# Spare products of ones and the identity at the start of a windowed attention, and masks made in two parts

## The reference, cut to what is computed

```python
def _attn_ref(q, k, v, n_global, n_local):          # q, k, v: 4 x 8 x 768 x 64
    scores = scale * np.matmul(q, k.transpose(0, 1, 3, 2))
    is_global = pos[None, :] < int(n_global)         # 8
    is_local = (rel >= 0) & (rel < int(n_local))     # 96
    dist = np.where(is_global & ~is_local, float(n_local), np.abs(rel))
    scores = scores - slopes[:, None, None] * dist   # a slope per head
    scores = np.where(is_global | is_local, scores, -1e9)
    a = softmax(scores)
    return np.matmul(a, v)
```

## Time and profile before

| what | us |
|---|---|
| median of three runs | 505.05 (504.94 to 505.18) |
| the profiled execution's own time | 504.66 |
| span of its instructions, first to last | 502.9 |
| TensorE busy | 479.9, or 95% of the span |
| VectorE busy | 363.8, or 72% |
| ScalarE busy | 346.6, or 69% |
| GpSimd busy | 94.4, or 19% |

### The profile page before, as it was taken

The page is one execution under the profiler, slowest core; times in us unless marked ns, Lnnn a source line. Parts: engine busy times, 40 slices in busy tenths (PEclk is TensorE's granted clock), DMA queues, the critical chain, the costliest instruction groups (busy, mean ns, idle before and its releaser), DMA issues.

```text
span 502.9 us, 12848 instructions
## 1 busy us (share of the span) xinstructions
PE 479.9 (95%) x4604; PEld 398.6 (79%) x4604; DVE 363.8 (72%) x1026; ACT 346.6 (69%) x763; POOL 94.4 (19%) x223
## 2 busy tenths in 40 slices
PE   2999999999999998998899999999999999999996
PEld 1667777677676642426689999999999999999996
DVE  5687877786787571318998978777587777768782
ACT  2788897887888710008999877777777776777740
POOL 1545554554455404400000000000000000000000
PEclk9999999999999999999999999999999999999999
DMA  7699889885565789994001011010110101001011
GB/s 284 256 343 366 343 316 328 322 299 195 175 200 195 296 327 405 417 404 162 1 1 44 2 43 42 0 42 0 42 42 0 42 0 42 28 14 42 0 43 42
DMA packets 17979, 77.24 MB, mean 154 GB/s; under 512 B 2320, under 2 KB 2320, under 8 KB 14352
## 3 DMA queue, kind: packets, MB, share of 16 engines
q1 hardware_dynamic: 14720, 60.95, 32.8%
q10 hardware_dynamic: 3216, 15.73, 8.2%
HBM read 70.39 MB, written 6.29 MB: 152 GB/s over the span
## 4 chain that ended last, share of the span: by engine, by line
PE 76%; ACT 9%; DVE 4%; DMA 3%; issue 3%; SPq 2%; POOL 1%; DVEq 0%; ACTq 0%; POOLq 0%
PE bank L1652 14%; PE bank L1651 14%; PE bank L1653 14%; PE bank L1308 5%; ACT probs L1028 5%; PE bank L1623 4%; PE bank L1296 4%; PE bank L1323 4%; DMA w_a<-w_dram 2%; PE bank L1328 2%; SPq L413 2%; PE bank L1291 2%; PE bank L1369 2%; PE bank L1580 2%; PE bank L1348 2%
## 5 line engine op out<-in xcount | busy, mean ns | idle before, releaser
L1028 ACT ACTIVATE probs<-probs,nmax 128x232 f32<-128x232 f32 (+1 forms) x192 | 88.6, 463 | 31.1 <-DVE nmax L554 30.2
L464 POOL TENSOR_SCALAR probs<-probs,rden 128x232 f32<-128x232 f32 (+1 forms) x192 | 82.5, 448 | 89.0 <-DVE rden L563 89.0
L1651 PE MATMUL bank<-t_hi,s_hi 128*128 128x256 f32 x352 | 98.7, 280 | 0.0
L1652 PE MATMUL bank<-t_lo,s_hi 128*128 128x256 f32 x352 | 98.6, 280 | 0.0
L1653 PE MATMUL bank<-t_hi,s_lo 128*128 128x256 f32 x352 | 98.5, 280 | 0.0
L1151 ACT ACTIVATE g_s<-bank 128x1024 f32<-128x1024 f32 x47 | 47.9, 1022 | 29.2 <-PE bank L1623 29.2
L1199 ACT ACTIVATE s_hi<-s 128x512 fp32r<-128x512 f32 x88 | 55.0, 627 | 18.5 <-DVE s L956 14.7
L1651 PEld LDWEIGHTS bank<-t_hi,s_hi 128*128 128x128 f32 x352 | 66.5, 189 | 0.0
L1652 PEld LDWEIGHTS bank<-t_lo,s_hi 128*128 128x128 f32 x352 | 66.4, 189 | 0.0
L1653 PEld LDWEIGHTS bank<-t_hi,s_lo 128*128 128x128 f32 x352 | 66.4, 189 | 0.0
L879 DVE TENSOR_TENSOR s_lo<-s,s_hi 128x512 fp32r<-128x512 f32 x88 | 56.9, 687 | 6.8 <-DVE s L956 3.5
(11 more groups left out here) (200 smaller groups left out, 1024.2 us busy)
## 6 DMA issues: line engine op xcount, KB each, us to landing
qkv_s<-qkv_dram SPq DMA_DIRECT2D x15, 1028.0 KB, 7.3
qkv_s<-qkv_dram SPq DMA_DIRECT2D x16, 704.0 KB, 5.9
w_s<-w_dram ACTq DMA_DIRECT2D x5, 2048.0 KB, 11.4
w_s<-w_dram SPq DMA_DIRECT2D x13, 512.0 KB, 8.6
out_dram<-o_stage SPq DMA_DIRECT2D x24, 256.0 KB, 2.0
wo_raw<-w_out_dram SPq DMA_DIRECT2D x4, 1024.0 KB, 14.5
w_a<-w_dram SPq DMA_DIRECT2D x3, 1024.0 KB, 11.6
w_a<-w_dram SPq DMA_DIRECT2D x5, 512.0 KB, 7.5
```

The lines of the kernel that those rows point to most:

```text
L464: last = pool.tensor_scalar(probs[:, v % 2, m, a, 0:w], probs[:, v % 2, m, a, 0:w], rden[:, v % 2, m, a:a + 1], 1.0, ALU.mult, ALU.mult)
L1028: act.activation(probs[:, v % 2, m, a, 0:w], probs[:, v % 2, m, a, 0:w], ACT.Exp, bias=nmax[:, v % 2, m, a:a + 1], scale=-1.0, accum_out=d ...
L1651: pe.matmul(OUT[n], hi, W_HI[n](at_f), start=(c == 0 and f == 0 and n in (0, 2, 4, 5)), stop=False, skip_group_check=True)
L1652: pe.matmul(OUT[n], hi, W_LO[n](at_f), start=False, stop=False, skip_group_check=True)
```

## The change

The first tile's masks of heads 0 and 1 are made as soon as the first tile's tables stand, and `bias_scores(0, 0)` is split: tile `m` = 0 is masked before the tables and masks of the other tiles are made, tile `m` = 1 after. The masks of later heads move by one step: those of head s + 1 are made after step s, for s from 1 to 6. TensorE gets products of `ones` and `ident` into a part of bank 7 that nobody reads: 12 before its step 0 (after a wait for the identity, which before stood behind step 0), 4 behind step 0 and 22 behind step 1.

```diff
-                own(dve.tensor_scalar(drop[:, at_g], col[:, 0:GLOB], ng, masked, ALU.is_ge, ALU.mult))
-                own(dve.scalar_tensor_tensor(drop[:, :], rel[:, :], nl, drop[:, :], ALU.is_ge, ALU.mult))
-                own(dve.tensor_scalar(dist[:, :], rel[:, :], nl, None, ALU.min))
-
-                def make_bias(h):
+
+                def make_bias0(h):
 
                     slope = 2.0 ** (-8.0 * (h + 1) / HEADS)
                     dve.scalar_tensor_tensor(bias0_of(h), dist0[:, :], -slope / SCALE, drop0[:, :], ALU.mult, ALU.add)\
                         .then_inc(masks_ready, 1)
+
+                def make_bias(h):
+
+                    slope = 2.0 ** (-8.0 * (h + 1) / HEADS)
                     dve.scalar_tensor_tensor(bias_of(h), dist[:, :], -slope / SCALE, drop[:, :], ALU.mult, ALU.add)\
                         .then_inc(masks_ready, 1)
 
-                for h in range(2):
-                    make_bias(h)
-
-                def bias_scores(b, v):
+                def bias_scores(b, v, tiles=(0, 1)):
                     p, i0 = divmod(2 * v, TILES)
-                    for m in range(2):
+                    for m in tiles:
...
-                for s in range(STEPS):
-
-                    dve.wait_ge(masks_ready, 2 * min(s + 2, HEADS))
+                for h in range(2):
+                    make_bias0(h)
+                dve.wait_ge(masks_ready, 2)
+                bias_scores(0, 0, (0,))
+                own(dve.tensor_scalar(drop[:, at_g], col[:, 0:GLOB], ng, masked, ALU.is_ge, ALU.mult))
+                own(dve.scalar_tensor_tensor(drop[:, :], rel[:, :], nl, drop[:, :], ALU.is_ge, ALU.mult))
+                own(dve.tensor_scalar(dist[:, :], rel[:, :], nl, None, ALU.min))
+                for h in range(2):
+                    make_bias(h)
+                dve.wait_ge(masks_ready, 4)
+                bias_scores(0, 0, (1,))
+                recips(0, 0)
+                for s in range(1, STEPS):
+                    dve.wait_ge(masks_ready, 2 * min(s + 1, HEADS))
                     step(0, s, False)
-                    if s + 2 < HEADS:
-                        make_bias(s + 2)
+                    if s + 1 < HEADS:
+                        make_bias0(s + 1)
+                        make_bias(s + 1)
...
+            def idle_start(n):
+
+                for _ in range(n):
+                    pe.matmul(bank[7][:, 0:P], ones[:, :], ident[:, :])
+
             if windowed:
+                pe.wait_ge(iotas, 6)
+                idle_start(12)
                 for s in range(STEPS):
                     step(0, s, False)
-                    if s == 0:
-                        pe.wait_ge(iotas, 6)
+                    if s < 2:
+                        idle_start((4, 22)[s])
```

## The result

The changed kernel takes 511.67 us (median of 6 runs, 511.27 to 513.75) against 505.12 (504.81 to 505.88) for the kernel before: a ratio of 1.0139, 95% interval 1.0127 to 1.0152. The medians are 6.55 us apart. The profiled execution took 511.46, its span 509.7 against 502.9, so 6.8 us of difference are there to be read. The forecast was 509.7 with a range of 507.8 to 512.8. The direction and the range held. The place of the loss was the one named, but the likeliest case, with its own range of 508.9 to 510.5, was not the one that came: TensorE's clock fell after the gap, the rival given 0.25. The range held because it had been drawn wide enough for that rival.

The account below looks back on a forecast made before the run. At the start, whichever engine each step waits for bounds the kernel: TensorE for step 2, then VectorE's loop. 4.5 us (step 2) plus 0.15 (later masks) gives 4.7, so 509.3 profiled, 509.7 median; range 507.8 to 512.8.

Parts of the forecast that it names:

- the likeliest case: The main forecast, chance 0.58: TensorE's clock stays up and the time is 509.7 us, own range 508.9 to 510.5.
- the rival given 0.25: TensorE's clock falls while idle between step 1's scores and step 0's transposes: 1.9 to 2.8 us more, 511.6 to 512.5.
- Part 1, the 12 products: Ahead of step 0: 24 records from 2.40 us, clock rising at 7.3, hold up the scores; tile 0 masked at 8.4.
- Part 2, the masks: Step 0 on VectorE: other tiles' tables and masks stand behind the wait for TensorE; sums arrive at 12.4 against 11.38.
- d: Delay of step 0's sums from the held-up scores and new mask order: 1.1 us, bounds 0.65 to 2.0.
- Part 3, the 4 products: Behind step 0 on TensorE: 0.9 us fast or 1.7 slow, hidden because VectorE wants step 1's scores only at 12.9.
- Part 4, the 22 products: Between step 0's transposes and step 2's scores: 44 records, 4.9 us; step 2 masked at 21.4, 4.5 us late.
- the two bursts: TensorE work from 5.26 and 12.89 us in the kernel before, read as bounding the clock's rise to 3.9 to 5.9 us.
- Part 5, later masks: Step 6 gains a pair of masks, step 0 loses one: 0.15 us before step 7, bounds 0 and 0.35.
- The products did not pass the waiting transposes: Rival, chance 0.08: TensorE runs the 22 products in the gap, ahead of the waiting transposes: 503.8 to 504.8 us.
- Nothing was taken up later: Rival, chance 0.04: a wait in the loop hides the delay, time within 0.2% of 505.05 us.
- The clock did rise early: Rival, chance 0.05, claimed the opposite: first products too little to raise the clock, d 2.0, 22 products slow: 512.9 us.

Follow-up runs that it names:

- masks_alone: The changed kernel with its new mask order and none of the added products: 504.66 us, ratio 0.9999 to the kernel before.
- no_22: The changed kernel without the 22 products behind step 1: 505.90 us, ratio 1.0016 to the kernel before.
- only_22: The kernel before, old masks, with only the 22 products behind step 1 added: 510.45 us, ratio 1.0112 to the kernel before.
- twice_22: The changed kernel with 44 products in place of 22 behind step 1: 516.22 us, ratio 1.0220 to the kernel before.
- gap_filled: The changed kernel with 12 more products between step 1's scores and step 0's transposes: 508.98 us, ratio 1.0088 to the kernel before.
- old_masks_12_4: The kernel before, old masks, with 12 products ahead of step 0 and 4 behind it: 504.54 us, ratio 0.9992.
- fill_old: The kernel before, old masks, with 10 products ahead of step 0, 4 behind it, 8 before step 0's transposes: 504.53 us, ratio 0.9986.
- fill_new: The changed kernel with 8 products ahead of step 0, 4 behind it, 12 before step 0's transposes, no 22: 504.38 us, ratio 0.9983.

## Why the prediction was right, and where it was off

Step 2 was to come at 21.4 and came at 23.53; the sum to there was 4.5 and is 6.63.

- **Part 1, the 12 products.** Right, and late within its bounds. The steps were 0.213 us and the last of the 24 records began at 7.48, but the scores began only at 7.83: 0.35 us after the last product's start where a step of 0.21 had been counted, and the clock rose at 8.3, the late bound, not 7.3. Tile 0 was masked at 9.13 instead of 8.4.
- **Part 2, the masks.** Right in the mechanism: the tables of the other tiles stood behind the wait. The term from tile 0 to tile 1 measured 2.30 and not 2.52, since the gap of 0.22 us after the last mask was 0.03. So d was 1.58 at the sums, 1.45 at the transposes, for a forecast of 1.1. masks_alone shows that without products, and so without a fast clock, the new order costs and brings nothing that can be measured.
- **Part 3, the 4 products.** Right: the scores of step 1 ended at 11.0 and were wanted at 13.43.
- **Part 4, the 22 products.** The mechanism is right and carries the result: no_22, only_22 and twice_22 each show it. The step that failed is the choice that the clock stays up over the gap. The four transposes took 0.91 instead of 0.44 us, the 44 records 6.18 instead of 4.93, some 12 of them slow (1.25 us at 0.10 each). gap_filled shows that idleness is the cause. Its price as a rival had been 1.9 to 2.8; it measured 0.47 + 1.25 = 1.7. The clock was back at 18.6, 4.2 us after the burst began at 14.34, and so within the 3.9 to 5.9 of the two bursts. But the rival's sum had counted these from the second tile's transposes (13.75) and not from the first tile's (12.89), where the burst begins: 0.86 us, or 4 slow records, too many. From the first tile's it gives 10 to 19 slow records and 1.4 to 2.3 us.
- The scores, 1.24 us to VectorE's start, were as forecast (1.2). Sum of the misses: 0.35 (d) + 0.47 + 1.25 + 0.04 = 2.1, which is 6.63 - 4.5.
- **Part 5, later masks.** 6.78 - 6.63 = 0.15 at step 7, as forecast; that the rest of the program passes the shift on is right too: 6.78 to 6.81 from step 7 to the end of the attention, 6.8 at the end of the span.
- **Rivals.** The one given 0.25 came. The products did not pass the waiting transposes: their 44 records stand behind them. Nothing was taken up later. The clock did rise early, so that rival falls.

That the clock would fall with idle gaps is what the Trainium skill, "TensorE: Matmul & The Clock Gate", section "Why this matters for your kernels", says; the traces agree for the gap of 3.33 us, and show the fall after 2.48 us too, a gap shorter than those that the page warns of. I had put more weight on the kernel's own trace, which held no gap of the kind once the clock was up. A trace without an example was no evidence for the clock staying up. The same page's Part 4, that transposes stay at the lower clock, is contradicted again: 0.44 us for two transposes at 14.34, and 0.66 for four in gap_filled, against 1.12 slow.

## What to carry to other kernels

Filling products belong where TensorE waits, ahead of the wait that ends the gap, and not between the last thing that was waited for and the next thing that is wanted; each one behind the wait is paid in full, here 0.22 us a product at the upper clock and 0.43 at the lower. An early clock that falls again in the next gap gained nothing that can be measured here (old_masks_12_4); with the gap filled step 2 came 0.95 us earlier than that in the trace, but the two kernels' times do not differ (504.53 and 504.54 us). Before warming an engine, read which engine sets the next step: here, with the old masks, at most 0.9 us could be had before VectorE's own loop took over. The best version gained 0.7 to 0.9 us, less than one later load's issue varied between executions (3.47 to 4.98 us).

## What was not expected of the hardware

- The clock fell after idle stretches of TensorE of 3.33 us (the change, no_22) and already of 2.48 us (old_masks_12_4). The fall need not come in the gap: it came 0.4 to 0.9 us after work had begun again in these three, and at 12.7 us, inside a gap that ended at 13.19, in twice_22. It did not after idle pieces of 0.4 to 0.8 us (gap_filled, fill_old, fill_new).
- The rise comes at different times in different executions of nearly the same start. Products began at 2.41 us each time; the first scores behind 24 records began at 7.83 (the change), 7.43 (old_masks_12_4), 7.14 (gap_filled) and 6.91 us (twice_22), the earlier the more records ran fast. In no_22 the clock, down again after the gap, was still low at 19.31, where eight transposes took 1.97 us in place of the change's 1.09. After a gap the clock was back 4.2 us after work began again in the change, 4.3 in old_masks_12_4, 6.3 in twice_22 and 7.3 in no_22; the bound of 3.9 to 5.9 from the two bursts of the kernel before does not hold for all of them.
- The granted clock is printed as 1.00 before its first record, though the instructions there run at half pace.
